# The second expert product by 128 + 96 rows, with four 32-column matmuls side by side, in a kernel of attention and two expert layers

## What is computed

```python
attn_out = attention(q, k, v, cap)        # 4 batches, 12 heads, 448 positions, 64 wide; capped by tanh
x = attn_out as [1792, 768]
x = square(max(x @ w_in, 0)) @ w_out      # 768 -> 2048 -> 768
# 8 experts, each takes exactly 224 of the 1792 rows (greedy by gate logit)
for e in range(8):
    h = np.maximum(x[mask_e] @ w1[e], 0.0)   # [224, 768] @ [768, 1024]
    out[mask_e] = h @ w2[e]                  # [224, 1024] @ [1024, 768]
```

## Time and profile before

| | |
|---|---|
| median of 3 runs | 1069.16 us (1068.51 to 1069.37) |
| profiled execution, its own time | 1069.24 us |
| its span | 1067.3 us |
| mean granted clock of TensorE | 0.989 of 2.4 GHz |
| TensorE (PE) busy | 1030.2 us, 97% of the span |
| VectorE (DVE) busy | 819.7 us, 77% |
| ScalarE (ACT) busy | 588.9 us, 55% |
| GpSimd (POOL) busy | 197.3 us, 18% |
| expert stage | from about 797 us to the end |

### The profile page before, as it was taken

How to read it: one execution, slowest core, us unless ns; L and a number is a source line. 1 busy time by engine, 2 the same in 40 slices (tenths; PEclk the granted TensorE clock), 3 DMA queues, 4 the chain that set the end, 5 groups by cost and what they waited for, 6 DMA issues and landing times.

```text
span 1067.3 us, 23613 instructions
## 1 busy us (share of the span) xinstructions
PE 1030.2 (97%) x8724; PEld 752.5 (71%) x8724; DVE 819.7 (77%) x1699; ACT 588.9 (55%) x942; POOL 197.3 (18%) x319
## 2 busy tenths in 40 slices
PE   6999999999999999999999999999987999999996
PEld 3444444444469999999976666666656889888895
DVE  5899999999968656665686667666678899999971
ACT  5888888989846233333461111313215688877791
POOL 3444444444310000000000000000001132212211
PEclk9999999999999999999999999999997999999998
DMA  3752211121033000000241040401048566677401
GB/s 93 206 143 60 65 55 52 52 60 52 19 128 119 2 1 2 2 2 1 89 150 31 16 149 16 149 16 31 16 148 276 181 234 233 248 269 286 158 14 52
DMA packets 66782, 103.44 MB, mean 97 GB/s; under 512 B 14480, under 2 KB 44432, under 8 KB 66704
## 3 DMA queue, kind: packets, MB, share of 16 engines
q1 hardware_dynamic: 64144, 91.34, 26.0%
q0 software_dynamic: 2560, 11.01, 3.4%
HBM read 91.32 MB, written 11.01 MB: 96 GB/s over the span
## 4 chain that ended last, share of the span: by engine, by line
PE 84%; DVE 9%; issue 4%; ACT 1%; DMA 1%; POOL 0%; SPq 0%; DVEq 0%; POOLq 0%; ACTq 0%
PE psum L1465 21%; PE psum L1652 17%; PE psum L1760 10%; PE psum L1746 9%; PE psum L1510 6%; PE psum L1495 6%; PE psum L1519 5%; PE psum L1655 3%; DVE arena L1030 2%; PE psum L1685 2%; PE psum L1542 1%; PE psum L1728 1%; PE psum L1581 1%; DVE arena L1364 1%; DVE arena L1354 1%
## 5 line engine op out<-in xcount | busy, mean ns | idle before, releaser
L1465 PE MATMUL psum<-arena 128*128 128x224 f16 x2304 | 224.4, 259 | 1.6 <-DVE arena L1002 1.0
L1465 PEld LDWEIGHTS psum<-arena 128*128 128x128 f16 x2304 | 219.8, 98 | 6.1 <-issue 3.2
L1652 PE MATMUL psum<-arena 128*128 128x384 f16 x1152 | 195.9, 326 | 0.0
L1652 PEld LDWEIGHTS psum<-arena 128*128 128x128 f16 x1152 | 107.7, 98 | 66.8 <-issue 0.8
L590 POOL TENSOR_SCALAR arena<-arena 128x448 f32<-128x448 f32 x168 | 105.5, 639 | 160.9 <-DVE arena L1012 160.9
L1760 PE MATMUL psum<-arena 128*112 128x384 f16 x768 | 127.1, 326 | 0.4 <-issue 0.4
L723 ACT ACTIVATE arena<-arena 128x448 f32<-128x448 f32 x168 | 125.6, 750 | 1.0 <-DVE arena L1032 1.0
L805 ACT ACTIVATE arena<-psum,arena 128x384 f32<-128x384 f32 x28 | 16.3, 581 | 186.5 <-PE psum L1652 144.3
L1746 PE MATMUL psum<-arena 128*128 128x224 f16 x1152 | 114.5, 262 | 3.8 <-DVE arena L1390 2.0
L1760 PEld LDWEIGHTS psum<-arena 128*112 128x112 f16 x768 | 99.3, 130 | 24.8 <-issue 0.8
L1746 PEld LDWEIGHTS psum<-arena 128*128 128x128 f16 x1152 | 111.9, 99 | 6.2 <-DVE arena L1390 2.4
(11 more groups left out here) (238 smaller groups left out, 1389.4 us busy)
## 6 DMA issues: line engine op xcount, KB each, us to landing
arena<-moe_w SPq DMA_DIRECT2D x16, 3072.0 KB, 11.7
arena<-moe_w_out SPq DMA_DIRECT2D x32, 384.0 KB, 3.9
arena<-moe_w_in SPq DMA_DIRECT2D x16, 384.0 KB, 4.5
arena<-q SPq DMA_DIRECT2D x24, 224.0 KB, 2.7
arena<-v SPq DMA_DIRECT2D x24, 192.0 KB, 2.4
arena<-k SPq DMA_DIRECT2D x24, 96.0 KB, 2.6
arena<-k SPq DMA_DIRECT2D x48, 48.0 KB, 2.3
y_rows<-arena SPq DMA_DIRECT2D x4, 336.0 KB, 2.4
```

The source lines that it names most:

```text
L1465: last = pe.matmul(out, w_split[:, f, z, k * 128:(k + 1) * 128], x[u % 2][:, k, :], start=(k == 0 and m == 0), stop=(k == KD - 1 and m == 2))
L1652: last = pe.matmul(psum[:, BANK_Y + q % 4, 0:HALF], g_pair(p)[:, x, k, i * 128:(i + 1) * 128], w_split[:, k, z, columns], **flags)
```

## The change

An expert's 224 rows are taken as 128 + 96 instead of 112 + 112 (tables, gather, transposes and scatter follow). The down jobs are cut anew. Jobs 2 and 3 are for the first 128 rows, one half of the outputs each. Jobs 0 and 1 are for the other 96 rows, with four matmuls at a time whose stationary operand has 32 columns and whose results go to four groups of 32 partitions of one bank. Job 0 takes rows 128 to 191 for both halves of the outputs (24 groups of four). Job 1 takes rows 192 to 223, both halves, and the 24 terms are dealt to two groups each, which gives 12 groups of four and two partial sums. ScalarE reads out one partial sum (`s_op`) and VectorE adds the other to it (`rows_sum`); this addition, and no longer the eviction, makes job 1's bank free (`s_o`). `turn_rows` goes ahead of the down jobs, `rows_hi` behind the fourth ReLU, and `rows_lo` ahead of the maximum of h. The scatter takes the 96 rows first.

```diff
@@ gather and scatter (GpSimd)
-                    pool.indirect_dma_start(out=yg[0:TP, c, :], out_offset=None, in_=y_d[:, :],
+                    pool.indirect_dma_start(out=yg[0:SLOTS[c], c, :], out_offset=None, in_=y_d[:, :],
...
-                for c in range(2):
+                for j, c in ((1, 1), (3, 0)):
                     if expert_live(e):
-                        hold(s_o, 4 * e + 2 * c + 4)
+                        hold(s_o, 4 * e + j + 3)
@@ ScalarE
                     if j == 0 and not is_last(e) and not first(e):
                         w2_hi(e, 2, 3)
+                    if j == 3 and not first(e + 2) and not first(e + 1):
+                        rows_hi(e + 2)
                     if j > 0 and not first(e + 1):
                         w2_abs(e + 1, j - 1)
...
                         wait(act, s_free, e + 1)
-                        act.activation(e_out[0:TP, j // 2, (j % 2) * (DM // 2):(j % 2 + 1) * (DM // 2)],
-                                       psum[0:TP, BANK_E2 + j % 2, 0:DM // 2], ACT.Copy, scale=o_inv[0:TP]).then_inc(s_o, 1)
+                        if j == 2:
+                            wait(act, s_o, 4 * e + 4)
+                        source = psum[:, BANK_E2 + j % 2, 0:HALF]
+                        if j >= 2:
+                            act.activation(e_out[:, 0, (j % 2) * HALF:(j % 2 + 1) * HALF], source, ACT.Copy, scale=o_inv).then_inc(s_o, 1)
+                            return
+                        rows = slice(0, 64) if j == 0 else slice(64, 96)
+                        for n in range(2):
+                            part = slice(64 * n, 64 * n + 64 - 32 * j)
+                            last = act.activation(e_out[rows, 1, n * HALF:(n + 1) * HALF], source[part], ACT.Copy, scale=o_inv[part])
+                        last.then_inc(s_o if j == 0 else s_op, 1)
...
                     w1_hi(e + 2, 2)
-                    rows_hi(e + 2)
                     w1_hi(e + 2, 3)
@@ VectorE
+                def rows_sum(e):
+                    wait(dve, s_op, e + 1)
+                    for n in range(2):
+                        part, rows = slice(64 * n + 32, 64 * n + 64), e_out[64:96, 1, n * HALF:(n + 1) * HALF]
+                        last = dve.scalar_tensor_tensor(rows, psum[part, BANK_E2 + 1, 0:HALF], o_inv[part], rows, ALU.mult, ALU.add)
+                    last.then_inc(s_o, 1)
+
                 def up_lo(e):
                     for j in range(3):
+                        if j == 2 and expert_live(e - 2):
+                            rows_sum(e - 2)
                         w1_lo(e, j)
...
-                    rows_lo(e)
                     w1_lo(e, 3)
...
                 if is_last(e):
                     rows_scale(e)
+                    rows_sum(e)
...
                 elif expert_live(e + 1):
+                    if expert_live(e + 2):
+                        rows_lo(e + 2)
                     wait(dve, s_ER, 4 * (e + 2) + 2)
                     dve.tensor_reduce(eh_max, eh, AX.X, ALU.max).then_inc(s_em, 1)
...
                         w2_scale(e + 1)
+                    if is_last(e + 1):
+                        rows_sum(e)
@@ TensorE
             def expert_down(e, j):
-                c, half = j // 2, j % 2
                 wait(pe, s_eL, 2 * (e + 1))
                 wait(pe, s_w2L, 4 * (e + 1))
                 wait(pe, s_o, 4 * e + j + 1)
+                pe.sem_inc(s_pe, 1)
...
-                for k in range(KE):
-                    cols = slice(half * (DM // 2), (half + 1) * (DM // 2))
-                    for m, (h, w) in enumerate(((hh, wH), (hh, wL), (hl, wH))):
-                        last = pe.matmul(psum[0:TP, BANK_E2 + j % 2, 0:DM // 2], h[:, k, c * TP:(c + 1) * TP], w[:, k, cols],
-                                         start=(k == 0 and m == 0), stop=(k == KE - 1 and m == 2))
+                terms = [(k, h, w) for k in range(KE) for h, w in ((hh, wH), (hh, wL), (hl, wH))]
+                half = len(terms) // 2
+                out = psum[:, BANK_E2 + j % 2, 0:HALF]
+                if j >= 2:
+                    for t, (k, h, w) in enumerate(terms):
+                        last = pe.matmul(out, h[:, k, 0:FULL], w[:, k, (j % 2) * HALF:(j % 2 + 1) * HALF],
+                                         start=(t == 0), stop=(t == 2 * half - 1))
+                for t in range((2 * half, half)[j] if j < 2 else 0):
+                    for group in range(4):
+                        n, r = group // 2, group % 2
+                        k, h, w = terms[t + half * r * j]
+                        first_slot = FULL + 32 * (2 if j else r)
+                        last = pe.matmul(out[32 * group:32 * group + 32], h[:, k, first_slot:first_slot + 32], w[:, k, n * HALF:(n + 1) * HALF],
+                                         start=(t == 0), stop=(t == (2 * half, half)[j] - 1))
                 last.then_inc(s_E2, 1)
...
                     expert_up(e + 1)
+                if expert_live(e + 2) and not first(e + 1):
+                    turn_rows(e + 2)
                 if expert_live(e):
                     expert_down(e, 0)
                     expert_down(e, 1)
-                if expert_live(e + 2) and not first(e + 1):
-                    turn_rows(e + 2)
-                if expert_live(e):
                     expert_down(e, 2)
                     expert_down(e, 3)
```

More of the change, by code:

```diff
@@ L54 @@
 QK_ROWS = (TP, 128)
+FULL = 128
+SLOTS = (FULL, CAP - FULL)
 BEHIND = 2
@@ L139, in build @@
         grid = lambda: take(CH * E).rearrange("p (c e) -> p c e", e=E)
+        group_hot = view(at[0], CH * CH).rearrange("p (c g) -> p c g", c=CH)
+        assert CH * CH <= 2 * CH * E
         masked, best, pick, newly, place = grid(), grid(), grid(), grid(), grid()
@@ L153, in build @@
         at[0] = X_ODD
-        low_hot = take(CH * TP // 2, F16).rearrange("p (c q) -> p c q", c=CH)
-        group_hot = take(CH * CH).rearrange("p (c g) -> p c g", c=CH)
+        low_hot = take(CH * FULL // 2, F16).rearrange("p (c q) -> p c q", c=CH)
         group_tok = take(CH * CH // 2, F16).rearrange("p (c g) -> p c g", c=CH)
@@ L172, in build @@
         groups, tok = take(CH), take(CH)
-        lows = take(TP)
-        grid_i = take(TP, I32)
+        lows = take(FULL)
+        grid_i = take(FULL, I32)
         tok_i = take(CH, I32)
@@ L277, in build @@
         s_E1, s_ER, s_em, s_ea, s_ee, s_eH, s_eL = sem("expert_up"), sem("expert_relu"), sem("eh_max"), sem("eh_amax"), sem("eh_scale"), sem("eh_hi"), sem("eh_lo")
-        s_E2, s_o, s_oi, s_idx, s_sct, s_free = sem("expert_down"), sem("out_rows"), sem("out_inv"), sem("out_index"), sem("out_written"), sem("out_rows_free")
+        s_op = sem("out_rows_part"); s_E2, s_o, s_oi, s_idx, s_sct, s_free = sem("expert_down"), sem("out_rows"), sem("out_inv"), sem("out_index"), sem("out_written"), sem("out_rows_free")
         s_wgl = sem("gate_loaded")
@@ L602, in _ @@
             pool.iota(w8_i.bitcast(I32), [[-1, E]], base=E, channel_multiplier=0).then_inc(s_rt, 1)
-            pool.iota(grid_i, [[1, TP]], base=0, channel_multiplier=0).then_inc(s_rt, 1)
+            pool.iota(grid_i, [[1, FULL]], base=0, channel_multiplier=0).then_inc(s_rt, 1)
             pool.iota(tok_i.rearrange("p (b c) -> p b c", b=B)[0:TP], [[S, B], [1, NC]], base=0, channel_multiplier=NC).then_inc(s_rt, 1)
@@ L643, in gather_rows @@
                 hold(s_tT, 3 * e)
-                pool.tensor_copy(row_idx[0:TP], ids[0:TP, bass.ds(2 * e, 2)]).then_inc(s_gidx, 1)
+                pool.tensor_copy(row_idx, ids[:, bass.ds(2 * e, 2)]).then_inc(s_gidx, 1)
                 hold(s_gidx, e + 1)
@@ L649, in gather_rows @@
                 for c in range(2):
-                    pool.indirect_dma_start(out=yg[0:TP, c, :], out_offset=None, in_=y_d[:, :],
-                                            in_offset=bass.IndirectOffsetOnAxis(ap=row_idx[0:TP, c:c + 1], axis=0)).then_inc(s_ygl[c], 16)
+                    pool.indirect_dma_start(out=yg[0:SLOTS[c], c, :], out_offset=None, in_=y_d[:, :],
+                                            in_offset=bass.IndirectOffsetOnAxis(ap=row_idx[0:SLOTS[c], c:c + 1], axis=0)).then_inc(s_ygl[c], 16)
             def step(e):
@@ L668, in step @@
                 if expert_live(e):
-                    pool.tensor_copy(idx[0:TP], ids[0:TP, bass.ds(2 * e, 2)]).then_inc(s_idx, 1)
+                    pool.tensor_copy(idx, ids[:, bass.ds(2 * e, 2)]).then_inc(s_idx, 1)
                     hold(s_idx, e + 1)
-                for c in range(2):
+                for j, c in ((1, 1), (3, 0)):
                     if expert_live(e):
-                        hold(s_o, 4 * e + 2 * c + 4)
-                        pool.indirect_dma_start(out=out_d, out_offset=bass.IndirectOffsetOnAxis(ap=idx[0:TP, c:c + 1], axis=0),
-                                                in_=e_out[0:TP, c, :], in_offset=None).then_inc(s_sct, 16)
+                        hold(s_o, 4 * e + j + 3)
```

(18 more changed lines are left out.)

## The result

The changed kernel takes 1102.46 us (median of 4 runs, 1100.76 to 1103.91), the kernel before 1069.26 in the same comparison: a ratio of 1.0311, 95% interval 1.0299 to 1.0323. It is slower by 33 us; 1101 was forecast. The profiled execution has a span of 1099.0 us.

The account below looks back on a forecast made before the run. TensorE bounds the old kernel; the change makes job 3 wait for VectorE's addition. 1069.2 + 19.0 (3.2 step 0, 11.2 periods, 4.2 end, 0.4 tables) + 12.6 clock gives 1101 us, range 1092 to 1109, 1086 to 1109 with rival (a).

Parts of the forecast that it names:

- TensorE's own work: Per expert, jobs 0 and 1 cost 6.06 us; down falls by 1.74 to 13.86, TensorE alone needing 28.82.
- rival (d): 32-column matmuls in jobs 0 and 1 are bound by weight loads: 1104, up to 1140 us; chance 0.04.
- The addition: rows_sum on VectorE, two 384-element operations from PSUM ahead of w1_lo part 2, adds 1.14 us per expert.
- When job 3 can start: Job 3 waits for VectorE's addition until T + 28.9, T being the start of expert_up; TensorE idles 4.0 us.
- The ring without the clock: VectorE's run, addition, job 3 and eviction form a loop: 32.8 us per expert, +19.0 in all, 1088.2 us.
- The clock: Seven TensorE stalls, before job 3 of experts 0 to 5 and the last expert_down, lose 1.8 us each: 12.6.
- rival (a): The ring is as told, but the clock holds through the stalls: 1088 us; chance 0.12.
- The end: Expert 6's addition delays expert 7's low part of h; last expert_down at T + 35.9 instead of 30.0, net +4.2 us.
- The tables and the last scatter: Tables of 128 instead of 112 columns and a last scatter of 128 rows: +0.4 us, bounds 0 and 1.
- The moves save nothing: The earlier turn and rows_lo gain nothing, since what they make ready earlier is not what is late.
- Rival (b): TensorE stays the bound, the addition being done before job 3 needs it: faster, 1056 us; chance 0.06.
- Rival (c): VectorE only carries 1.14 us more per expert, and job 3 does not wait: about 1072 us; chance 0.04.

Follow-up runs that it names:

- the last experiment: On top of quarters with a bank of its own, rows_lo and the scale of w2 put into VectorE's gaps behind GpSimd's reductions; 1062.06 us, 0.9936.
- addition earlier: Changed kernel with the addition ahead of w1_lo part 0 instead of part 2, and rows_out(1) ahead of w1_hi part 1; 1078.60 us, 1.0094.
- the filled kernel: Changed kernel with useless matmuls put into TensorE's idle time ahead of job 3 and ahead of the last expert_down; 1088.80 us, 1.0189.
- old order: Changed kernel with rows turned between jobs 1 and 2 again, and rows_hi, rows_lo back behind w1_hi and w1_lo part 2; 1087.02 us, 1.0165.
- quarters: Changed kernel with job 1's four groups each taking a quarter of the outputs and all 24 terms, without partial sums or rows_sum; 1065.60 us, 0.9972.
- quarters with a bank of its own: On top of quarters, job 1 in its own PSUM bank, and the last expert's w2 high parts ahead of rows_out(1); 1065.09 us, 0.9964.
- own bank: Changed kernel with job 1 in a separate PSUM bank, so job 3 no longer waits for the addition, which stays; 1079.76 us, 1.0105.

## Why the prediction was right

- **TensorE's own work** (6.06 for jobs 0 and 1, 28.82 in all): 5.97 in the changed kernel, and 28.85 between the starts where nothing else binds, in the last experiment. Two small errors cancel in it by luck: jobs 0 and 1 cost 0.09 less than the 6.06, and the turn 1.25 us (950.12 to 951.37) instead of 1.16. The 32-column matmuls run four abreast, so rival (d) is out.
- **The addition** (1.14): 1.28 from its start to the next `w1_lo`. Each operation is 618 ns, close to the slope's 610. The pair takes 1.25, so the second did not start 0.08 us before the first ended, as the prediction had it.
- **When job 3 can start** (T + 28.9): T + 29.1 in four of the five steady periods, 29.3 in the first. The idle time is 4.0, as forecast (4.03 in the trace, which counts it from the 4.07 us of job 2; 4.2 by the prediction's own count with 3.90). That this wait is a cause and not a mere companion is shown twice: with another bank for job 1 it goes, with the addition earlier in the queue it shrinks, and the time falls by 23 and 24 us though VectorE does the same work.
- **The ring without the clock** (32.8 per expert, 1088.2 in all): 33.0 and 1088.8 in the kernel whose idle time is filled. In its profiled run, 0.7 over the median, the parts are 4.1 for step 0 (forecast 3.2), 12.5 for the five periods (11.2) and 3.9 for the end with tables and scatter (4.6): 20.5 against 19.0, so part of the close match in the total is luck.
- **The clock** (1.8 at each of seven stalls, 12.6): for experts 0 to 5, the time from the start of job 3 to the next `expert_up` was 1.34 to 2.92 us longer than the 3.90 at full clock, 1.8 in the mean. Jobs 0 and 1 of the last `expert_down` took 7.18 instead of 5.97, 1.2 more. That is 12.1 by the trace; the filled kernel is 13.7 faster by the medians and 11.25 by the two profiled executions. The term had been bounded from 0 to 2.8 and its middle was a choice, so that it was met so well is partly luck, and one stall (2.92) lies above the upper bound.
- **A stall that the prediction did not list:** TensorE also waits 3.17 us for the addition ahead of job 3 of expert 6, and that job is busy 5.74 us instead of 4.06. It costs nothing, since the last `expert_down` waits for something else: it starts at T + 36.1 in the filled kernel too, where that job is not slowed.
- **When the clock falls:** the prediction read a fall 1.4 us into an idle time and set it against rival (a). Its row was of an idle time of 8.05 us behind a few 16-column matmuls, and in the stalls of the changed kernel no fall came so early: before job 3 of expert 2 the engine had been idle from 925.5, and the clock fell within the microsecond from 928. The Trainium skill ("TensorE: Matmul & The Clock Gate", HAM oscillation) has the engine start cold behind such a gap in every turn. The trace agrees in that all six turns ran part of job 3 at the lower clock, but not in that the start is always cold: ahead of job 3 of experts 3 and 6 the clock was 1.00 when the job started, and fell 0.7 and 1.3 us later, estimates from the mean clock of 0.59 and 0.79 in the microseconds from 966 and 1068.
- **The end** (T + 35.9 to the last `expert_down`): 1076.30 - 1040.19 = 36.1.
- **The tables and the last scatter** (0.4, by size): not seen. From the end of the last matmul to the end of the span are 7.6 us (1091.45 to 1099.0), where they were 8.0 (1059.29 to 1067.3).
- **The moves save nothing**: shown for the kernel before (no difference). In the changed kernel they cost 15 us, as `rows_lo` lies ahead of the addition: 1.5 us in each of six turns of the ring, and most of the rest since the clock falls less behind shorter gaps (8.4 us lost with the old order, against 12.1, by the same count).
- Rival (a), the clock holds, is what the filled kernel is. Rival (b), TensorE stays the bound, needed more than a free bank: VectorE stood ready as the next bound, at 31.5 us per expert with the addition and 30.0 without. Rival (c) is close to the experiments with another bank and with the early addition, 1080 and 1079: its 1072 left out the end, where the addition of expert 6 still holds back the low part of h, and the clock in the last `expert_down`.

## What to carry to other kernels

Before putting a small operation on a second engine's queue, work out when that queue reaches it and what the main engine has queued behind it: 1.25 us of addition made a wait of 4.0 because 24 us of other work stood ahead of it. A saving on the bound engine is worth only the distance to the next one, here 0.5 us per expert of the 1.7 (30.04 against 30.56) until VectorE's own waits were filled too. Cutting the output instead of the sum (quarters) gave the same packing and nothing to add up.

## What the runs showed that I had not expected

The clock's cost came on top at every turn of the ring, and filling the gap with matmuls that nobody reads gained 13.7 us. Between 2.1 and 3.2 us the length of the gap did not decide. Gaps that were followed by the lower clock: 2.12 us (quarters with a bank of its own, ahead of the last `expert_down`), 2.13 (own bank, at 931.18), 2.31 (quarters, job 3 of expert 6), 2.53 (old order). Gaps that were not: 2.13 (VectorE's gaps used, ahead of the last `expert_down`), 2.43 (old order), 2.51 and 3.16 (addition earlier, job 3 of experts 0 and 6):

```profile
1044.28 4.06 PE L1789 MATMUL psum<-arena 128*128 128x384 f16 x24 [3.16 <-DVE arena L1396]
```

All gaps of 4.0 us and more in the loop and behind it brought the clock down, none under 2.0 did. Groups of four with 192 moving columns were no dearer per column than groups with 384.
